# Choosing an expert's tokens by a search in five digits of 6, 6, 6, 7 and 7 bits instead of six of 5, 5, 5, 5, 6 and 6

## What is computed

```python
def _moe2_ref(x, w_gate, w1, w2):
    N, D = x.shape                  # 2304, 512
    E = w_gate.shape[1]             # 8
    cap = N // E                    # 288
    flat = (x @ w_gate).flatten()
    order = np.argsort(-flat)
    ...
    for idx in order:
        tok, e = (int(idx) // E, int(idx) % E)
        if assigned[tok] >= 0 or counts[e] >= cap:
            continue
        assigned[tok] = e
        counts[e] += 1
    ...
    for e in range(E):
        mask = assigned == e
        h = np.maximum(x[mask] @ w1[e], 0.0)
        out[mask] = h @ w2[e]
    return out
```

## Time and profile before

| | |
|---|---|
| median of 3 runs | 875.1 us (873.21 to 876.34) |
| profiled execution: its own time | 873.38 us |
| its span, first to last instruction | 871.6 us |
| mean granted TensorE clock | 0.971 |
| PE, PEld, DVE busy | 825.1 (95%), 749.6 (86%), 508.0 (58%) us |
| ACT, POOL busy | 406.6 (47%), 333.4 (38%) us |

### The profile page before, as it was taken

One profiled execution on the slowest core, in us unless ns is written; L12 is line 12 of the kernel. 1 busy time (PEld: TensorE's weight loads), 2 busy tenths in 40 slices (PEclk: granted clock), 3 DMA queues, 4 the chain that ended last, 5 costly groups with the idle time before them and its releaser, 6 DMA issues. The chain is left out here.

```text
span 871.6 us, 21161 instructions
## 1 busy us (share of the span) xinstructions
PE 825.1 (95%) x7658; PEld 749.6 (86%) x7658; DVE 508.0 (58%) x1424; ACT 406.6 (47%) x1006; POOL 333.4 (38%) x391
## 2 busy tenths in 40 slices
PE   6979999999999999999999999939999999999995
PEld 5867888888889888888898989838999999999995
DVE  4667766655665665563534344366766766766620
ACT  4655555444535544553444444303454455455461
POOL 6661133203302321340000000007687786787882
PEclk8899999999999999999999999967999999999998
DMA  9975421320321233201101000006625625616611
GB/s 203 251 191 143 142 68 41 96 80 21 86 80 45 68 87 80 66 2 39 49 2 49 0 24 1 13 13 221 212 62 197 228 58 207 228 47 219 219 39 45
DMA packets 99301, 85.49 MB, mean 98 GB/s; under 512 B 63664, under 2 KB 71856, under 8 KB 99248
## 3 DMA queue, kind: packets, MB, share of 16 engines
q1 hardware_dynamic: 93808, 74.74, 29.5%
q0 software_dynamic: 3072, 9.44, 3.7%
q10 hardware_dynamic: 2368, 0.59, 0.4%
HBM read 70.60 MB, written 14.16 MB: 97 GB/s over the span
## 5 line engine op out<-in xcount | busy, mean ns | idle before, releaser
L528 PE MATMUL PS<-xs,W 128*128 128x256 f32 x1728 | 234.0, 285 | 1.3 <-DVE xT L432 1.3
L528 PEld LDWEIGHTS PS<-xs,W 128*128 128x128 f32 x1728 | 222.5, 189 | 12.4 <-issue 3.3
L528 PE MATMUL PS<-W,g 128*128 128x512 f32 x864 | 223.9, 396 | 5.4 <-DVE g L669 5.0
L528 PEld LDWEIGHTS PS<-W,g 128*128 128x128 f32 x864 | 152.4, 188 | 37.4 <-DVE g L669 9.6
L633 ACT ACTIVATE scratch<-PS,minus 128x256 f32<-128x256 f32 x144 | 68.3, 474 | 218.4 <-DVE scratch L660 218.4
L660 DVE TENSOR_SCALAR scratch<-PS 128x256 f32<-128x256 f32 x144 | 60.9, 423 | 124.9 <-PE PS L528 124.4
L441 POOL TENSOR_TENSOR P<-P,top 128x640 f32<-128x640 f32 x11 | 13.9, 1262 | 224.4 <-DVE top L391 224.4
L1539 POOL TENSOR_TENSOR w1s<-w1r,w1s 128x512 fp32r<-128x512 f32 x64 | 80.9, 1291 | 29.1 <-ACT w1s L1427 28.8
L1334 PE MATMUL PS<-exs,w1s 128*128 128x288 f32 x256 | 81.1, 317 | 0.0
L1334 PE MATMUL PS<-ehs,w2s 128*128 128x288 f32 x256 | 80.9, 316 | 0.0
L1335 PE MATMUL PS<-exs,w1s 128*128 128x288 f32 x256 | 76.1, 297 | 0.0
(11 more groups left out here) (198 smaller groups left out, 1449.8 us busy)
## 6 DMA issues: line engine op xcount, KB each, us to landing
w1r<-in_moe_w SPq DMA_DIRECT2D x16, 1024.0 KB, 5.0
w2r<-in_moe_w SPq DMA_DIRECT2D x16, 1024.0 KB
vd<-in_v SPq DMA_DIRECT2D x16, 288.0 KB
xt<-xT SPq DMA_DIRECT2D x16, 288.0 KB, 2.2
y<-scratch SPq DMA_DIRECT2D x18, 256.0 KB, 2.1
vw<-in_v SPq DMA_DIRECT2D x34, 128.0 KB, 2.8
scratch<-in_moe_w_in SPq DMA_DIRECT2D x8, 512.0 KB, 6.1
scratch<-in_moe_w_out SPq DMA_DIRECT2D x8, 512.0 KB, 5.4
```

Source lines behind the costliest of these rows:

```text
L528: r = pe.matmul(psum, wsel(w[i]), xsel(x[j]), start=first and t == 0, stop=last and t == 2)
```

## The change

The 32 bits are cut in five digits instead of six, so every choice has one chain of compare, count and sum less, and the compares have 64, 64, 64, 128 and 128 thresholds instead of 32, 32, 32, 32, 64 and 64. `COUNT`, `SUM`, their forms for round 0 and `SPLIT` get new values. `slot` (the numbers 1 to 96) is read from the first row of `thr`, which holds 1 to 128, and loses its own tensor and its POOL instruction.

```diff
-BITS = (5, 5, 5, 5, 6, 6)
+BITS = (6, 6, 6, 7, 7)
...
-                                ("slot", [128, GP], F32),
...
-                                               (con["slot"], [[1, GP]], 1, 0), (con["three"], [[1, GT]], 0, 0),
+                                               (con["three"], [[1, GT]], 0, 0),
...
-        thr, slot = con["thr"], con["slot"]
+        thr = con["thr"]
+        slot = thr[:, 0, 0:GP]
...
-        COUNT = [49, 55, 61, 3, 10, 19]
-        SUM = [51, 58, 63, 5, 13, 20]
-        COUNT_FIRST = [0, 0, 4, 9, 15, 21]
-        SUM_FIRST = [0, 0, 5, 10, 16, 22]
+        COUNT = [50, 58, 2, 11, 21]
+        SUM = [52, 61, 4, 13, 22]
+        COUNT_FIRST = [0, 0, 5, 13, 21]
+        SUM_FIRST = [0, 0, 6, 15, 22]
...
-                spans = sorted(set((TILES * k, (TILES - 1) * k + 128) for k in RADIX))
+                spans = sorted(set((TILES * k, (TILES - 1) * k + 128) for k in RADIX if k < 128))
...
-KEY_CHAIN, CHAIN = 5, 34
-CLEARED = 3 + len(set(RADIX))
+KEY_CHAIN, CHAIN = 5, 24 + 2 * (DIG - 1)
+CLEARED = 3 + len(set(k for k in RADIX if k < 128))
...
-SPLIT = 3
+SPLIT = 2
```

More of the change, by code:

```diff
@@ L974, in _ @@
                 dve_chunk(dve, MIXED, PLAN[0:1])
-                dve.wait_ge(con_ready, 7)
+                dve.wait_ge(con_ready, 6)
                 for i in range(1, DIG):
```

## The result

The changed kernel takes 882.67 us (median of 4, 881.88 to 885.05) against 875.06 us before (median of 4, 873.21 to 876.34). The ratio is 1.0104, with a 95% interval of 1.0087 to 1.0121: slower by 1% (9.1 us; the two medians are 7.6 us apart), where 884.2 us were predicted within 877.3 to 887.5. Its profiled execution is the slowest of the four, 885.05 us with a span of 883.0, so the two profiles differ by more than the medians. Of the difference between the spans, 11.4 us, 2.44 us lie in the untouched dense layers: choice 0 begins at 571.95 instead of 569.51 us in its timeline. Distances inside the third layer are therefore compared, not absolute times.

What follows compares the result with a forecast made beforehand. Rounds were taken as PE's and DVE's search plus a DMA-fixed stretch. 1.80 + 1.20 + 0.52 + 6 x 1.05 = 9.82 us on 873.38 gave 883.2, set at 884.2 as median; own range 881.5 to 887, full range 877.3 to 887.5.

Steps and rivals of the forecast that it cites:

- piece B: Round's last sum to next first transpose: fixed at 18.6 to 18.8 us by loads and gather sharing DMA; change 0.
- The compare: DVE's compare with 128 thresholds, 2304 elements: 2.56 us on the line through two rows, 2.62 in two parts.
- Choice 0: Search with nothing beside its chain: one digit less does not pay, longer compares add more; +1.8 us.
- Choice 1 ahead of the rounds: Digits 0 and 1 compare 64 thresholds instead of 32, 0.60 each, both waited for: +1.2 us, bounds 0.6 and 1.2.
- rival of a longer half clock: First expert matmuls: longer gaps put off PE's full clock, +1.4 us on top, 885.6 as a median; chance 0.12.
- Piece A in round 0: First transpose to last sum: count and sum saved, waits for longer compares added; +0.52 us, bounds -0.8 and +0.8.
- Piece A in the later intervals: First transpose to last sum, six intervals: count saved, last sum later, new waits; +1.05 us each, bounds 0.25 and 1.4.
- the gather is not held by the loads: Rival on piece B: it ends 3.27 us after the third gather's issue, 17.78 us; total 878 as a median; chance 0.22.

Runs made afterwards that it cites:

- after_gw: The changed kernel, with SP holding each w2 load from the second expert on until PE's first transposes of the gathered rows: 876.88 us, ratio 1.0036.
- late_sum: The kernel before, with only the last digit's count moved from step 19 to 21 and its sum from 20 to 22: 878.94 us, ratio 1.0058.
- warm6: The changed kernel with 6 instead of 14 idle warm-up matmuls ahead of the first count of choice 1: 883.28 us, ratio 1.0098.
- wide_rounds: The kernel before, with the two 64-threshold compares done 128 wide inside the rounds only, copies unused: 886.63 us, ratio 1.0146.
- before_gw: The kernel before, six digits, with SP holding the w2 load until PE's first transposes of the gathered rows: 871.59 us, ratio 0.9974.
- the hold: Edit to several kernels: SP issues w2 only after PE's first transposes of the gathered rows; ratio 1.0036 against 1.0104 on the changed kernel, 0.9974 on the kernel before.
- late_load: The kernel before, with DVE writing the chosen expert's number for SP three steps later, so w1's load starts 1.9 us later: 888.27 us, ratio 1.0191.
- late_load_gw: The kernel before, with the expert's number written 1.9 us later and w2 held until the first transposes: 873.51 us, ratio 0.9992.
- split3: The changed kernel, five digits, with three instead of two taken a round early and new COUNT and SUM places: 874.3 us, ratio 1.0003.
- split3_gw: The changed kernel with three digits taken a round early, new COUNT and SUM places, and w2 held until the first transposes: 870.62 us, ratio 0.9972.
- split3b_gw: As split3_gw, with the two wide digits counted at 7 and 16 instead of 8 and 18, summed at 8 and 17: 878.75 us, ratio 1.0053.

## Why the prediction was right, and where it was not

The time was inside the forecast's own range, with one term wrong in its mechanism. That the sum came out is in part luck: the ledger under piece B shows which errors met.

**The compare** (2.56 us expected) took 2.557, and 2.62 in two parts.

**Choice 0** (+1.8): from the first compare to the line behind the last kstar it is 590.48 - 574.07 = 16.41 us, to be set beside 14.65 of before (571.63 to the same operation at 586.28 in its timeline): +1.76.

**Choice 1 ahead of the rounds** (+1.2): too much in this profile. Expert matmuls begin 607.27 - 571.95 = 35.32 us after choice 0, against 602.25 - 569.51 = 32.74, so +2.6 in all and +0.8 for this term. The same distance was 31.65 to 34.13 us over the six-digit kernels whose early part was left alone and 34.91 to 36.10 over the five-digit ones, so 1.2 stays possible; single executions differ by more than the question. Part of it is the clock: the half clock at the first expert matmul was full in after's profile, while its warm-up matmuls had run at half. The rival of a longer half clock did not come about in that execution. It did in after_gw's profiled one: half clock from the first expert matmul at 605.85 to between 610 and 611 us, against 602.25 to between 605 and 606 in before's, and piece A of round 0 took 14.51 us instead of after's 12.87. How often that happens in unprofiled executions is not known.

**Piece A in round 0** (+0.5): the profile has 620.14 - 607.27 = 12.87 against 615.65 - 602.25 = 13.40, less and not more, because before's first dozen matmuls ran at half clock. In late_sum's profile, at full clock and with a last sum at step 22 in round 0 as before, it is 12.12. Against that one +0.75, inside the bounds.

**Piece A in the later intervals** (+1.05): 689.61 - 674.01 = 15.60 in after's profile, +1.33; 15.35 in those of warm6 and after_gw, +1.08 on 14.27. The terms hold, and wide_rounds shows that waits for compares are paid nearly in full. The 0.25 us in between are one digit's `full` again, 0.37 us later behind a count at the same place:

```profile
683.75 0.61 PE L1286 MATMUL PS<-hot,over 128*128 128x8 bf16 x18 [0.29 <-DVE over L1137]
684.77 0.17 DVE L1184 TENSOR_SCALAR full<-PS 128x8 bf16<-128x8 f32 x1 [0.71 <-PE PS L1286]
```

in after, and 682.14 - 681.50 = 0.64 us apart in after_gw. The sum term had no place for it.

**Piece B** (0): this is the step that failed. It said that the gather lands a fixed 16.5 us after w1's issue, so that from the last sum to the first transpose the time stays at 18.6 to 18.8. The runs showed two things in its place. Where the gather isn't late, B is PE's and DVE's, and it shrank to 18.3: in late_sum 0.43 of the 0.83 us by which the sum moved were given back. And where the load comes closer to the gather, as a last sum two steps later makes it, the gather is late by an amount that changes from round to round and from execution to execution (1.01 us in one interval of after's profile and none in the next; 0.7 to 1.4 in six of the seven rounds of warm6). What bounded the transposes of before, 0.1 to 0.3 us behind PE's arrival, was not that distance: in before_gw, where w2 is out of the way, they stand as far behind PE's arrival and behind the third gather (3.1 to 3.2 us). The two equal distances of 16.45 and 16.58 on which I leaned were a coincidence of a late gather in the one round and a punctual one in the other; the earlier trace rows already show it, with a wait of 0.63 us at the first and none at the second.

The forecast came out near the time because the two errors have opposite signs, which is luck. In the two profiles, from the start of choice 0 to the end, the ledger reads: ahead of the rounds +2.6 (forecast 3.0), A in round 0 -0.5 (+0.5), A in six intervals +7.8 (6.3), B in round 0 +0.3 and in six intervals -1.3 (0), the rest +0.1; together +9.0 against 9.8. The -1.3 of B is 0.4 us given back in each interval, 2.6 in six, less what the late gathers took. By the measured effect of the hold these took more in the other executions, nearly 6 us in the changed kernel and 2 in the kernel before, so some 4 of the change, give or take 2.5, against nothing in the forecast.

The rival "the gather is not held by the loads" was wrong as well: late_load and late_load_gw show that it is held, by w2, and B fell to 18.3 us and not to the rival's 17.8. With w2 out of the way it is the rival's 17.8 in round 0 (17.83 in after_gw) and still 18.3 in the later ones. The rule of the Trainium skill that it rested on ("DMA: Bandwidth & Descriptors", "Queues, rings and completion order") isn't refuted by this: taking turns between queues shares the engines and still makes the gather slower than alone. It doesn't say how late; the waits here are 0 to 2.8 us.

**Parts of the 1%.** With the hold on both kernels 5.3 us remain. In their profiles 3.8 of it lie between the first and the last of the seven first transposes (201.17 us against 197.36, 33.6 against 32.9 for one interval); the other 1.5, give or take 2, lies ahead of them. The rest of the ratio, 0.68% or 6 us, less the 2 us that the hold gives before too, goes with w2 beside the gathers. Why the hold gives after so much more than the 2.8 us that its profile showed is seen only in part; unprofiled executions have no waits to read.

## What to carry to other kernels

A search step that is hidden behind another engine's stream has a price only where it outlasts its steps, so fewer and longer steps must be placed anew, with room for everything else in that engine's order, before the saved step counts; placing alone moved this kernel by 1% either way (after against split3, split3_gw against split3b_gw). Ask of each transfer what else is in flight when a later schedule starts it: a load that started 1.9 us later cost 15 us here, since its second half then ran beside a small urgent gather, and with that half issued another 12 us later, behind the gather, the 15 us were gone. And two equal distances in a trace are no cause: delay the supposed cause alone and see whether the effect moves as far.

## What was not expected of the hardware

Three gathers of 96 rows each, 0.6 MB, are waited for by up to 2.79 us beside loads of 4 MB that the windows show at some 390 GB/s, and in the rounds by nothing without the second half of these. Rounds of one execution differ although w1 and the gathers are issued at the same distance: in after's profile w1 is issued 12.9 us ahead of the third gather in both the second and the third round, and the first transposes follow that gather by 674.01 - 669.75 = 4.26 us, waited for, and by 707.93 - 704.69 = 3.24. The trace's packet records show where the two rounds part: of the 2112 packets of the two loads all have ended 11.8 us after the first began in the third round, and in the second 25 are left at 12.0 us and the last ends at 14.4, beside the gather. In all rounds of before and after with a wait for the gather this train is 13.3 us or longer, and in all without one 12.8 or shorter. What makes the last one per cent late is open.

A DVE instruction that waits for PE's count starts 0.63 to 0.65 us behind the count's start in most digits, but 1.0 us in one digit of after and 1.3 and 1.5 us in two of split3b_gw, with DVE idle before it and in nearly every round of the execution.
